# Moving GpSimd's add and scale of a head pair, and one difference, to earlier tiles of the attention loop

## The reference

```python
q_bits = (einsum(q, proj) > 0); k_bits = (einsum(k, proj) > 0)
mask   = bucket(q_bits)[..., :, None] == bucket(k_bits)[..., None, :]
scores = where(mask, q @ k.T / 8, -1e9)
attn   = exp(scores - scores.max(-1)); attn /= attn.sum(-1) + 1e-9
x = attn @ v                               # 16 heads, to 1536 x 512
h = x @ w_in;  x = (h - tanh(h)) @ w_out    # 512 -> 2048 -> 512
out = sum over e of p[:, e] * (relu(x @ w1[e]) @ w2[e])   # 4 experts, 512 -> 1024 -> 512
```

## Time and the profile before

| what | value |
|---|---|
| median of 3 runs | 1031.46 us (1031.06 to 1031.79) |
| the profiled execution's own time | 1031.79 us |
| its span in the trace | 1029.9 us |
| TensorE busy | 999.4 us, 97% of the span |
| VectorE, ScalarE, GpSimd busy | 676.8, 463.6 and 418.5 us |
| mean granted TensorE clock, of full | 0.991 |

### The profile page before, as it was taken

One profiled execution on the slowest core, in us unless ns is written; L12 is line 12 of the kernel. 1 busy time (PEld: TensorE's weight loads), 2 busy tenths in 40 slices (PEclk: granted clock), 3 DMA queues, 4 the chain that ended last, 5 costly groups with the idle time before them and its releaser, 6 DMA issues.

```text
span 1029.9 us, 16517 instructions
## 1 busy us (share of the span) xinstructions
PE 999.4 (97%) x5438; PEld 921.3 (89%) x5438; DVE 676.8 (66%) x1129; ACT 463.6 (45%) x850; POOL 418.5 (41%) x424
## 2 busy tenths in 40 slices
PE   7999999899899999999979999999999999999998
PEld 5999998898899999999968888998998998988987
DVE  6888887788765546565858656556556555566554
ACT  4787778688444343443443322322233232322321
POOL 3676679986346264553630412203122121311200
PEclk9999999999999999999989999999999999999999
DMA  4465555462202002020010010101101020010003
GB/s 130 131 162 143 146 157 146 115 172 68 70 1 62 21 21 61 0 61 20 21 42 21 21 62 21 41 20 38 44 20 46 17 59 20 20 61 21 20 10 112
DMA packets 49525, 62.46 MB, mean 61 GB/s; under 512 B 5168, under 2 KB 31888, under 8 KB 49488
## 3 DMA queue, kind: packets, MB, share of 16 engines
q1 hardware_dynamic: 49328, 61.63, 20.8%
q10 hardware_dynamic: 160, 0.39, 0.1%
HBM read 44.07 MB, written 3.19 MB: 46 GB/s over the span
## 4 chain that ended last, share of the span: by engine, by line
PE 77%; POOL 7%; issue 7%; DVE 6%; ACT 2%; DMA 0%; POOLq 0%; ACTq 0%; SPq 0%; DVEq 0%
PE ps L1446 28%; PE ps L1469 25%; PE ps L1393 6%; PE ps L1363 5%; PE ps L1477 5%; PE ps L1374 5%; PE ps L1337 2%; POOL wu_lo L560 2%; POOL g_lo L628 2%; DVE xq_lo L1024 1%; DVE hb L1141 1%; ACT xq_hi L730 1%; DVE pT_lo L980 1%; ACT pT_hi L698 0%; DVE xq_raw L1012 0%
## 5 line engine op out<-in xcount | busy, mean ns | idle before, releaser
L1446 PE MATMUL ps<-xq_hi,wu_lo 128*128 128x384 f32 x672 | 228.9, 341 | 13.8 <-DVE xq_lo L1024 9.3
L1446 PE MATMUL ps<-xq_hi,wu_hi 128*128 128x384 f32 x672 | 227.2, 338 | 0.0
L1446 PE MATMUL ps<-xq_lo,wu_hi 128*128 128x384 f32 x672 | 227.1, 338 | 0.0
L560 POOL TENSOR_TENSOR wu_lo<-wu_raw,wu_hi 128x768 fp32r<-128x768 f32 (+1 forms) x48 | 106.6, 2235 | 259.6 <-ACT wu_hi L734 259.6
L1172 DVE SCALAR_TENSOR_TENSOR acc<-ps,p_norm,acc 128x512 f32<-128x512 f32 x180 | 135.1, 750 | 104.9 <-PE ps L1469 97.8
L1469 PE MATMUL ps<-wd_lo,g_hi 128*128 128x512 f32 x384 | 150.9, 393 | 0.0
L1469 PE MATMUL ps<-wd_hi,g_hi 128*128 128x512 f32 x384 | 150.9, 393 | 0.0
L1469 PE MATMUL ps<-wd_hi,g_lo 128*128 128x512 f32 x384 | 150.6, 392 | 0.0
L1446 PEld LDWEIGHTS ps<-xq_hi,wu_lo 128*128 128x128 f32 x672 | 126.8, 189 | 22.8 <-issue 11.0
L1446 PEld LDWEIGHTS ps<-xq_lo,wu_hi 128*128 128x128 f32 x672 | 127.0, 189 | 3.8
L877 ACT ACTIVATE g_hi<-hb 128x384 fp32r<-128x384 f32 x96 | 50.3, 524 | 177.1 <-DVE hb L1130 115.1
(11 more groups left out here) (120 smaller groups left out, 1747.8 us busy)
## 6 DMA issues: line engine op xcount, KB each, us to landing
wu_raw<-in_w SPq DMA_DIRECT2D x64, 128.0 KB, 2.4
wd_raw<-in_w SPq DMA_DIRECT2D x16, 512.0 KB, 3.4
q_raw<-in_qT SPq DMA_DIRECT2D x32, 192.0 KB, 3.2
k_raw<-in_kT SPq DMA_DIRECT2D x30, 192.0 KB, 3.3
wu_raw<-in_w_in SPq DMA_DIRECT2D x32, 128.0 KB, 2.2
wd_raw<-in_w_out SPq DMA_DIRECT2D x8, 512.0 KB, 3.5
v_raw<-in_vP SPq DMA_DIRECT2D x16, 192.0 KB, 2.8
inv_rows<-inv_dram SPq DMA_DIRECT2D x16, 192.0 KB, 3.3
```

What stands on the lines that cost most here:

```text
L560: rest = pool.tensor_tensor(wu[par][1][:, slots, :, :], wu_raw[:, slots, :, :], wu[par][0][:, slots, :, :].bitcast(F32), ALU.subtract)
L1446: mm = pe.matmul(to, w[:, wslot, k, :], x[:, xslot, k, :], start=start and k + m == 0, stop=k == 1 and m == 2, skip_group_check=not start)
```

## The change

Only GpSimd's order inside `pair` changes; no instruction is added or removed, and no other engine's program is touched.

- `x_add(it - 1)` moves from t = 6, behind `add_eps`, to t = 5, behind `k_rest` and so ahead of `add_eps`, in pairs 1 to 7.
- `x_scale(it - 1)` moves from t = 8, behind the value split, to t = 6, behind `add_eps` and ahead of the value split, in pairs 1 to 7.
- `x_sum(3)` moves from t = 9 to t = 8 of pair 4, ahead of `q_scale`.
- `x_sum(5)` moves from t = 7 of pair 5 to t = 9 of pair 4.

```diff
                             if not first:
                                 add_eps(h - 1, 1 - b)
                             if later and b == 1:
-                                x_add(it - 1)
+                                x_scale(it - 1)
                         if qt == 1:
                             v_round(h, b)
                             v_rest(h, b)
...
                         if qt == 5 and not last:
                             q_rest(h + 2, b)
                             k_rest(h + 2, b)
-                        if later and t == 8:
-                            x_scale(it - 1)
-                        if isinstance(it, int) and it == KT and t == 9:
-                            x_sum(3)
+                        if later and t == 5:
+                            x_add(it - 1)
+                        if isinstance(it, int) and it == KT and t in (8, 9):
+                            x_sum(3 if t == 8 else 5)
                         if isinstance(it, int) and it == KT + 1:
...
                             if t == 3:
                                 x_rest(0)
-                            if t == 7:
-                                x_sum(5)
```

## The result

| kernel | median us | lowest to highest | ratio to before, 95% interval |
|---|---|---|---|
| before | 1031.62 (4 runs) | 1031.06 to 1031.98 | |
| changed | 1037.61 (4 runs) | 1035.97 to 1039.28 | 1.0066 (1.0049 to 1.0084) |

The change costs 6.0 us; 6.3 were forecast (1037.8). The profiled execution of the changed kernel took 1036.07 us with a span of 1034.2, at the lower end of its runs. Why the runs differ is told under again1 to again3.

The account below looks back on a forecast made before the run. TensorE was taken to bound the kernel, so time is lost where late GpSimd work delays add_eps, the reciprocal and TensorE's transposes. Terms + 7.75 - 1.2 - 1.4 + 1.2 = + 6.35 us gave 1037.8 us, range 1033 to 1043.5.

Parts of the forecast that it names:

- GpSimd's spare time is of no use between release and reciprocal: Attention heads: GpSimd idles before TensorE's release (5.36 us in pair 2); afterwards a delay of add_eps reaches TensorE but for 0.24.
- x_add in pairs 1 to 4 and 6: x_add's 1.80 us ahead of add_eps, 0.24 hidden by pT_hi: 1.55 us a pair, 7.75 us in all.
- x_scale: Its 1.89 us moved ahead of the value split, hidden by GpSimd's idle time before the next q_round: cost 0.
- The differences in pair 4: x_sum(3) and x_sum(5) delay GpSimd 1.84 us, covered by TensorE's release coming 1.55 later: taken as 0, uncovered 1.84.
- Pair 5 and what follows its stall: Pair 5 relieved of x_sum(5): 1.2 us won; without its 3 us stall the clock stays up: 1.4 won in the next head.
- x_add in the last pair: Pair 7: x_add waits for its copy until 237.97, so pT_lo moves from 239.00 to 240.2: 1.2 us lost.
- The sum: Whole kernel: + 7.75 - 1.2 - 1.4 + 1.2 = + 6.35 us, forecast 1037.8 us.
- the likeliest case: The forecast itself, chance 0.65, said to span 1035.5 (pair 7 free, boundaries 1.3) to 1040 (boundaries 1.8, cover missing).
- A: Faster rival: TensorE doesn't feel the later reciprocal, only the relief in pairs 5 and 6 remains: 1028.9 us, chance 0.10.
- B: Slower rival: granted clock falls after three of seven TensorE pauses, 1.4 us each: 1042.0 us (all seven 1047.6), chance 0.15.
- C: Rival: delay partly won back inside the following head, some 0.75 us a boundary instead of 1.55: 1033.2 us, chance 0.10.

Follow-up runs that it names:

- again1: The changed kernel run once more, unaltered, for another trace; that execution took 1039.07 us.
- again3: The changed kernel run again, unaltered, for the last of three further traces; that execution took 1037.96 us.
- e6: Kernel before plus a GpSimd addition on a 128x640 buffer nobody reads, ahead of add_eps at each pair's other boundary: 1037.27 us, ratio 1.0057.
- e7: Kernel before plus a GpSimd addition on a 128x640 buffer nobody reads, right behind add_eps at each pair's other boundary: 1031.41 us, ratio 1.0001.
- e4_scale_alone: Kernel before with only x_scale moved from tile 8 to tile 6, ahead of the value split: 1031.27 us, ratio 0.9997.
- e1_add_back: Changed kernel with x_add put back behind add_eps at tile 6, the rest of the change kept: 1029.05 us, ratio 0.9977 to the kernel before.
- e3_sums_alone: Kernel before with only x_sum(3) and x_sum(5) moved, x_add and x_scale where they were: 1028.80 us, ratio 0.9973.
- e5_rests_later: e1_add_back with x_rest(3) also taken out of pair 5 and each later x_rest one place on: 1027.51 us, ratio 0.9965 to the kernel before.
- e8: Changed kernel with x_add put back behind add_eps in pair 7 alone: 1036.26 us, ratio 1.0042 to the kernel before.
- again4: The changed kernel unaltered, on the same chip and in the same rounds as e8: 1039.45 us, ratio 1.0069 to the kernel before.

## Why the prediction was right, step by step

**GpSimd's spare time is of no use between release and reciprocal: right.** e6 and e7 show it with an instruction that has nothing to do with the change: 6.0 us ahead of `add_eps`, 0.1 behind it.

**x_add in pairs 1 to 4 and 6, 1.55 us each: right.** The distance between the reciprocals of tile 6 of pairs 2 and 3 grew by 30.34 - 28.82 = 1.52 us. The wait on VectorE grew by 1.83 (0.38 to 2.21), and 0.24 of it was hidden by `pT_hi`, as reckoned. The copy was in time: the 0.24 us ahead of `x_add` in pair 2 is put down to `k_rest`, not to the copy, and `add_eps` had 0.17 of the same kind there before.

**x_scale, nothing: right** (e4_scale_alone, 1031.27 beside 1031.42).

**The differences in pair 4, nothing under cover of x_add's delay: right, and the cover is real.** In the changed kernel VectorE doesn't wait at that boundary; in e1_add_back, without the cover, it waits 1.33 us. Yet of the 1.84 us named for that case little is paid: in e1_add_back the head with the wait takes 1.4 us more and the next one 176.04 - 161.77 = 14.3 us instead of 15.5, so that 0.2 us is left over the two.

```profile
176.04 0.19 DVE L1031 RECIPROCAL inverse<-total_eps 128x6 f32<-128x6 f32 x1
```

e3_sums_alone has the same two moves, and the same two lengths to within 0.1 us. Why the next head is shorter, no run here shows.

**Pair 5 and what follows its stall, - 1.2 and - 1.4 us: right in kind, the sum somewhat too small.** From tile 6 of pair 5 to tile 6 of pair 6 the changed kernel took 3.0 us less, with pair 6's own 1.55 in it, so the relief is 4.5 us in this stretch by that estimate; pair 5's own delay was paid before it, 1.3 us by the distance from pair 4. Together they make - 3.2, where - 2.6 had been reckoned. The clock stayed up behind pair 5 in all five traces of the changed kernel, while in the kernel before it fell.

**x_add in the last pair, 1.2 us: the term that was mis-sized.** I took the copy's landing from the one profiled execution, in which `x_add` started at 237.97. (The row puts that wait down to TensorE, but the program has `x_add` wait for the copies alone.) The first trace of the changed kernel, with 3.0 us from issue to landing, has pair 7 1.4 us longer. Of that the last head gives 0.7 back, which the prediction, with its delay that isn't won back, left out. But in the four further traces the copy took up to 5.1 us, the reciprocal waited 2.78 to 3.58 us, and in two of them, with waits of 3.10 and 3.58, the clock fell behind it. Against the kernel before, pair 7 and the last head together took 0.7 us more in the first trace and 1.9 to 3.8 in those four. Where `x_add` stands behind `add_eps` most of the same lateness is hidden: in e5_rests_later, the fastest kernel, the copy's landing times (shortest, median, longest) were

```profile
DMA to landing us min/median/max: 3.0/3.3/4.9
```

and no reciprocal waited for it; the last head took 12.54 us there, against 12.41 in the kernel before. In e1_add_back and e3_sums_alone, with longest landings of 4.7 and 4.4 us, it took 13.02 and 12.69. By the medians of e8 and again4 the term is 3.2 us and not 1.2, by their means 2.7.

**The sum.** From the first reciprocal to tile 6 of pair 6 the five traces of the changed kernel took 4.3 to 4.8 us more than the kernel before, where 5.15 had been reckoned; pair 7 came out over its term in all but the first. So the agreement is partly luck: the median of the first four runs, 1037.61, agrees with 1037.8 in part because these errors offset each other. The median of 24 runs, 1038.2, lies 0.4 above it. The upper end of what the prediction calls the likeliest case is added up wrongly, too: with boundaries at 1.8 and the cover missing it is 1037.8 + 1.25 + 1.84 = 1040.9, not 1040.

**The rivals.** A (TensorE doesn't feel it) fell with the 1.82 us that TensorE's weight load waits and the 1.58 that TensorE itself idles in pair 2. Its number, 1028.9, is what e1_add_back and e3_sums_alone gave, 1029.05 and 1028.80, once `x_add` was out of the way. B (the clock falls behind the pauses) did not happen at the six boundaries of pairs 1 to 6, where TensorE idled 1.46 to 1.59 us. It happened in pair 7 in two of five traces, where TensorE idled 2.48 and 2.98 us; idle times of 0.99, 2.18 and 2.55 in the other three left the clock up. As 2.48 lowered it and 2.55 did not, the length of the pause alone doesn't decide; what else does, no run here shows. C (half is won back) fell with the distances in pairs 1 to 4, where 1.4 to 1.8 us a pair were paid; only in the last head did 0.7 us come back. The Trainium skill, page "TensorE: Matmul & The Clock Gate", section "A second HAM failure mode: psum-queue depth-cycling", has it that pauses that are short but frequent can make the clock swing. These traces don't show that for one pause of 1.5 to 1.6 us every 30 us.

## What to carry to other kernels

Look at an engine with much idle time for where the idle time lies: between the event that releases it and the result that others wait for, one more instruction costs most of its length (1.5 of 1.8 us a pair for `x_add`, 0.9 to 1.25 of 1.25 on VectorE's wait for the spare addition), and behind that result it is free. Work that itself waits for a transfer is a poor choice for such a place, as it hands the transfer's jitter (the variation of its landing time) on to the whole chain; a trace of one execution doesn't show that jitter. Where an engine is the bound in one pair only, moving extra work out of that pair can win more than the time by which the stall shrinks, as the clock can stay up behind it: e3_sums_alone shortened the stalled head by 1.75 us and the one behind it by 1.6.

## What the runs showed of the hardware that was not expected

- The copy of 192 KB inside SBUF landed 3.0 us after issue in one execution and 4.3 to 5.1 in four others of the same program, at the same place in it. In all five, four loads of 128 KB were issued 2 us behind it on the same queue, so the loads alone don't explain the difference; without them it wasn't tried. The other kernels show both as well: 4.4 to 4.9 in e1, e3 and e5, 3.0 to 3.3 in the other six.
- On GpSimd an addition of 128x640 float32 with one tensor as both inputs and output took 1.25 us in the median (once 2.28); one of 128x768 with two different inputs took 1.84. Scaled by the columns alone, an estimate from the 1.84, it would be 1.53. Which of the differences makes up the rest wasn't tried.
